# Attention and mixture of experts in one kernel: tile pairs of neighbouring tokens, first products moved into the attention's tail, second-layer tiles issued in pairs

## The reference

```python
scores = scale * np.matmul(q, k.transpose(0, 1, 3, 2))
x = (log1p(abs(i - j)) / log1p(max(i, 1)))[..., None]
bias = np.maximum(x @ w1 + b1, 0.0) @ w2
attn = softmax(scores + bias.transpose(2, 0, 1)[None])
x = np.matmul(attn, v)            # as (2304, 512)
P = np.exp(x @ w_gate - max)
for _ in range(8):
    P /= P.sum(1, keepdims=True) + 1e-09
    P /= P.sum(0, keepdims=True) + 1e-09
    P *= N / E
for e in range(E):
    out += P[:, e:e + 1] * (np.maximum(x @ moe_w1[e], 0.0) @ moe_w2[e])
```

## Time and profile before

| | before |
|---|---|
| median of 3 runs | 1900.03 us (1897.21 to 1900.62) |
| the profiled execution's own time | 1902.45 us |
| its span | 1900.7 us, mean granted clock 0.992 |
| PE busy | 1862.4 us (98%) |
| PEld / DVE / ACT / POOL busy | 1604.4 / 1069.7 / 769.3 / 1156.8 us |
| chain that ended last | PE 91%, DVE 4%, POOL 3%, issue 1% |

### The profile page before, as it was taken

How to read it: one execution, slowest core, us unless ns; L and a number is a source line. 1 busy time by engine, 2 the same in 40 slices (tenths; PEclk the granted TensorE clock), 3 DMA queues, 4 the chain that set the end, 5 groups by cost and what they waited for, 6 DMA issues and landing times.

```text
span 1900.7 us, 27972 instructions
## 1 busy us (share of the span) xinstructions
PE 1862.4 (98%) x10255; PEld 1604.4 (84%) x10255; DVE 1069.7 (56%) x1844; ACT 769.3 (40%) x1314; POOL 1156.8 (61%) x722
## 2 busy tenths in 40 slices
PE   8899999899899999999999999999999999999999
PEld 4677777588799888988898889888888988888888
DVE  8777777648645554457455544554465445544554
ACT  8777767433233333334333333333333333333331
POOL 7523225367666666666677666666666666666662
PEclk9999999899999999999999999999999999999999
DMA  7663551011122111111211111111121111111110
...
DMA packets 44164, 152.58 MB, mean 80 GB/s; under 512 B 9594, under 2 KB 18042, under 8 KB 29710
## 3 DMA queue, kind: packets, MB, share of 16 engines
...
...
## 4 chain that ended last, share of the span: by engine, by line
PE 91%; DVE 4%; POOL 3%; issue 1%; ACT 0%; DMA 0%; SPq 0%; DVEq 0%; POOLq 0%
PE banks L630 14%; PE banks L629 14%; PE banks L628 13%; PE banks L604 12%; PE banks L602 12%; PE banks L606 12%; PE banks L513 4%; PE banks L474 3%; PE banks L456 3%; POOL qk_hi L1167 3%; PE banks L457 2%; PE banks L539 1%; DVE x_lo L1004 1%; DVE h_lo L1081 1%; DVE total L1066 0%
## 5 line engine op out<-in xcount | busy, mean ns | idle before, releaser
L1194 POOL TENSOR_TENSOR w_lo<-stage,w_hi 128x1024 fp32r<-128x1024 f32 (+1 forms) x288 | 641.4, 2228 | 498.0 <-ACT w_hi L782 497.2
L602 PE MATMUL banks<-x_hi,w_hi 128*128 128x384 f32 x1344 | 452.2, 336 | 12.7 <-DVE u L1074 6.6
L630 PE MATMUL banks<-w_hi,h_lo 128*128 128x512 f32 x1152 | 458.4, 398 | 0.0
L629 PE MATMUL banks<-w_lo,h_hi 128*128 128x512 f32 x1152 | 455.9, 396 | 0.0
L604 PE MATMUL banks<-x_lo,w_hi 128*128 128x384 f32 x1344 | 454.2, 338 | 0.0
L606 PE MATMUL banks<-x_hi,w_lo 128*128 128x384 f32 x1344 | 450.7, 335 | 0.0
L628 PE MATMUL banks<-w_hi,h_hi 128*128 128x512 f32 x1152 | 448.5, 389 | 0.0
L820 ACT ACTIVATE h_hi<-corner 128x384 fp32r<-128x384 f32 x288 | 151.3, 525 | 691.5 <-DVE corner L1074 691.5
L1081 DVE SCALAR_TENSOR_TENSOR h_lo<-corner,h_hi 128x384 fp32r<-128x384 f32 x288 | 338.2, 1175 | 3.1
L1074 DVE TENSOR_TENSOR corner<-u,banks 128x384 f32<-128x384 f32 x288 | 158.3, 550 | 270.7 <-PE banks L606 270.3
L602 PEld LDWEIGHTS banks<-x_hi,w_hi 128*128 128x128 f32 x1344 | 254.0, 189 | 39.0 <-DVE x_lo L1004 9.7
...
## 6 DMA issues: line engine op xcount, KB each, us to landing
...
```

What stands on the lines that cost most here:

```text
L602: pe.matmul(dst, hi[:, w, f], x_hi[:, k, c, :], start=fresh and c == 0, stop=False, skip_group_check=not fresh)
L629: pe.matmul(dst, h_hi[:, g % 2, f, tokens], lo[:, f], start=False, stop=False)
L630: mm = pe.matmul(dst, h_lo[:, g % 2, f, tokens], hi[:, f], start=False, stop=fp == FPAIRS - 1 and f == 1)
L1194: pool.tensor_tensor(lo, of, hi.bitcast(F32), ALU.subtract).then_inc(w_split, 1)
```

## The change

- `x_block` takes tile 2p and its neighbour 2p + 1, so that the first pair is tokens 0 to 767; `out_rows` and `tile_weight` follow. `PIECES_0` falls from 45 to 42.
- ACT makes the rounded inputs of the first pair in the last attention steps (after steps 16, 18 and 19 of the last period and tail steps 0 to 3), and DVE their splits after steps 17 and 19, tail steps 0 to 2, and two behind the tail. ACT's rounding of group 1's weights gets a wait for the last values product. The last period of DVE's loop is written out.
- PE issues products 0 and 1 of group 0 after tail steps 0 and 4.
- The first `split_pair` goes from POOL to DVE, behind the bias stage's last instruction; ACT rounds its input after four bias tiles instead of before them; DVE's two copies for the second piece go behind attention steps 0 and 1. `qk_hi` and `k_lo` become separate tensors per slot, and the buffers of the expert stage get another order in memory (`x_lo` in two tensors).
- Second-layer tiles are issued as `TILES_AFTER`: 0 and 1 after product 1, 2 and 3 after product 3, 4 after product 5, 5 after product 6.
- `scale_first` runs one tile at a time in the `add_tile` places of group 7, not six in a row behind group 6; in a group before a new tile pair, the third combination (`corner[:, 2]`) comes ahead of `split_factor(p + 1, 2)`.

```diff
@@ -45,7 +45,10 @@
 ALL = TILE_PAIRS * PERIODS
 PRODUCTS = ((0, 0, True), (4, 1, True), (1, 0, False), (5, 1, False), (3, 0, True), (2, 1, True), (6, 0, False))
 NP = len(PRODUCTS)
+TILES_AFTER = ((), (0, 1), (), (2, 3), (), (4,), (5,))
+TAIL_PRODUCTS = {(0, 0): 0, (0, 1): 4}
 SUMS = 4
+EARLY = 3
 BLOCK = 2 * P
 RAW = 4 * BLOCK + 2 * DM
 STAGE = RAW + SUMS * BLOCK
...
@@ -132,8 +135,10 @@
             probs_t = eb("probs_t", [P, 2 * KC + 1, S])
             heads = eb("heads", [P, 2, S])
             raw = eb("raw", [P, 2, 2, 2, S])
-            qk_hi = eb("qk_hi", [P, 2, 2, 2, S], F32R)
-            k_lo = eb("k_lo", [P, 2, 2, S], F32R)
+            qk_hi, k_lo = [], []
+            for i in range(2):
+                qk_hi.append(eb(f"qk_hi{i}", [P, 2, 2, S], F32R))
+                k_lo.append(eb(f"k_lo{i}", [P, 2, S], F32R))
             bias = eb("bias", [P, QC, 2, S])
             v_main = eb("v_main", [P, 2, KC, 2 * D])
             v_rest = eb("v_rest", [P, 2, 2 * D])
...
@@ -221,7 +230,7 @@
 
         X_PIECES = PAIRS * B
         LAST = PAIRS * STEPS
-        PIECES_0 = PIECES * (X_PIECES - 1)
+        PIECES_0 = PIECES * (X_PIECES - 2)
         Y_BANK = 2
         LOGIT_BANK = Y_BANK + 3
         TURNED_BANK = Y_BANK + 5
...
@@ -253,7 +262,7 @@
 
         def x_block(p, half, part):
 
-            return x[:, 2 * half:2 * half + 2, part * (N // 2) + p * T:part * (N // 2) + p * T + T]
+            return x[:, 2 * half:2 * half + 2, (2 * p + part) * T:(2 * p + part) * T + T]
 
         def x_sum(p, i):
 
...
@@ -385,7 +397,7 @@
             pairs_of(PAIRS - 1, True)
 
 
-            out_rows = out.rearrange("(a t j p) d -> a t p j d", a=2, t=TILE_PAIRS, p=P)
+            out_rows = out.rearrange("(t a j p) d -> a t p j d", a=2, t=TILE_PAIRS, p=P)
             for g in range(2, ALL):
                 sp.wait_ge(w_split, NW * (g - 1))
                 load_weights(g)
...
@@ -562,10 +574,6 @@
             with pe.Fori(1, PAIRS) as hp:
                 for s in range(STEPS):
                     step(hp, s)
-            for s in range(TAIL):
-                step(PAIRS, s)
-
-
             def product(g, k):
 
                 w, which, fresh = PRODUCTS[k]
...
@@ -573,6 +581,8 @@
                 if g % PERIODS == 0:
                     pe.wait_ge(x_split, NP * p + k + 1)
                 if k == 0:
+                    if g == 0:
+                        pe.wait_ge(biased, 2 * LAST)
                     pe.wait_ge(w_split, NW * g + 2)
                     if g > 0:
                         pe.wait_ge(combined, 5 * g - 1)
...
@@ -601,11 +611,17 @@
                     f = slice(c * P, c * P + P)
                     pe.matmul(dst, hi[:, w, f], x_hi[:, k, c, :], start=fresh and c == 0, stop=False,
                               skip_group_check=not fresh)
-                    pe.matmul(dst, hi[:, w, f], x_lo[:, k, c, :], start=False, stop=False,
+                    pe.matmul(dst, hi[:, w, f], x_low(k)[:, c, :], start=False, stop=False,
                               skip_group_check=not fresh)
                     mm = pe.matmul(dst, lo[:, w, f], x_hi[:, k, c, :], start=False, stop=c == 1,
                                    skip_group_check=not fresh)
                 mm.then_inc(product_done, 1)
+
+            for s in range(TAIL):
+                step(PAIRS, s)
+                for (g, k), after in TAIL_PRODUCTS.items():
+                    if after == s:
+                        product(g, k)
 
             def second_layer(g, j):
 
...
@@ -681,10 +697,11 @@
                 for k in range(NP):
                     if g == 1 and k == 2:
                         turn_logits()
-                    if g < ALL:
+                    if g < ALL and (g, k) not in TAIL_PRODUCTS:
                         product(g, k)
-                    if g > 0 and k > 0:
-                        second_layer(g - 1, k - 1)
+                    if g > 0:
+                        for j in TILES_AFTER[k]:
+                            second_layer(g - 1, j)
                 if g == 0:
                     logits()
 
...
@@ -714,16 +731,16 @@
             def round_pair(n, slot, h):
 
                 act.wait_ge(raw_in[slot], 16 * (n - slot + 2))
-                act.activation(qk_hi[:, slot, :, h, :], raw[:, slot, :, h, :], ACT.Copy).then_inc(rounded, 1)
+                act.activation(qk_hi[slot][:, :, h, :], raw[:, slot, :, h, :], ACT.Copy).then_inc(rounded, 1)
 
             for m in range(AHEAD):
                 hidden_units(m, m, again=False)
-            for h in range(2):
-                round_pair(0, 0, h)
             act.wait_ge(shift_kept, 2)
             for m in range(ROUND):
                 hidden_units(m + AHEAD, (m + AHEAD) % ROUND, again=m + AHEAD >= ROUND)
                 keep_bias(m, m, again=False)
+            for h in range(2):
+                round_pair(0, 0, h)
             with act.Fori(1, BIAS_TILES // ROUND - 1) as i:
                 for slot in range(ROUND):
                     hidden_units(ROUND * i + slot + AHEAD, (slot + AHEAD) % ROUND)
...
@@ -772,6 +789,8 @@
 
                 if i == 0:
                     act.wait_ge(w_in[g % 2], 16 * (g // 2 + 1))
+                    if g == 1:
+                        act.wait_ge(pv_done, len(PV_PARTS) * X_PIECES)
                     if g > 1:
                         act.wait_ge(product_done, NP * (g - 1))
                 elif i == 1:
...
@@ -781,17 +800,11 @@
                 hi, _, of = weight_part(g, i)
                 act.activation(hi, of, ACT.Copy).then_inc(w_rounded, 1)
 
-            for s in range(STEPS):
-                step(PAIRS - 1, s, last=True)
-                if s in (7, 9, 14):
-                    round_weights(0, (7, 9, 14).index(s))
-            for s in range(TAIL):
-                step(PAIRS, s)
-
             def round_factor(p, k):
 
                 if p == 0:
-                    act.wait_ge(scores_ready, 2 * LAST)
+                    act.wait_ge(scores_ready, 2 * (LAST - QC))
+                    act.wait_ge(split_done, 2 * X_PIECES)
                     act.wait_ge(scaled, PIECES_0)
                 else:
                     act.wait_ge(product_done, NP * (PERIODS * p - 1) + k + 1)
...
@@ -799,6 +812,17 @@
                 if needed:
                     act.wait_ge(x_summed, SUMS * p + needed)
                 act.activation(x_hi[:, k], x_factor(p, k), ACT.Copy).then_inc(x_rounded, 1)
+
+            for s in range(STEPS):
+                step(PAIRS - 1, s, last=True)
+                if s in (7, 9, 14):
+                    round_weights(0, (7, 9, 14).index(s))
+                for k in {16: (0,), 18: (1,), 19: (2,)}.get(s, ()):
+                    round_factor(0, k)
+            for s in range(TAIL):
+                step(PAIRS, s)
+                if s < NP - EARLY:
+                    round_factor(0, EARLY + s)
 
             def keep_first(g):
                 act.wait_ge(product_done, NP * g + 1)
...
@@ -838,8 +862,6 @@
                 for j in range(2):
                     act.activation(to[:, :, 4 + j, :], second[:, :, C * j:C * j + E], ACT.Copy).then_inc(logit_ready, 1)
 
-            for k in range(NP):
-                round_factor(0, k)
             for g in range(ALL):
                 p, at = g // PERIODS, g % PERIODS
                 more = g + 1 < ALL
...
@@ -916,9 +938,11 @@
 
             dve.wait_ge(attn_consts_in, 32)
             dve.tensor_copy(select_r[:], select_in).then_inc(select_kept, 1)
-            for h in range(2):
-                dve.wait_ge(raw_in[1], 32)
-                dve.tensor_copy(qk_hi[:, 1, :, h, :], raw[:, 1, :, h, :]).then_inc(rounded, 1)
+            dve.wait_ge(rounded, 2)
+            dve.tensor_tensor(qk_hi[0][D:2 * D, 0, :, :], raw[D:2 * D, 0, 0, :, :],
+                              qk_hi[0][D:2 * D, 0, :, :].bitcast(F32), ALU.subtract).then_inc(split_done, 1)
+            dve.tensor_tensor(k_lo[0][:, :, :], raw[:, 0, 1, :, :], qk_hi[0][:, 1, :, :].bitcast(F32),
+                              ALU.subtract).then_inc(split_done, 1)
 
             def keep_heads(hp, s, half):
 
...
@@ -990,19 +1014,31 @@
                             dve.tensor_copy(probs_t[:, 2 * KC, q_at:q_at + rows],
                                             rest_bank[:, 0:rows]).then_inc(kept_t[2], 1)
 
+            def split_factor(p, k):
+                dve.wait_ge(x_rounded, NP * p + k + 1)
+                if p == 0 and k == EARLY:
+                    dve.wait_ge(scores_ready, 2 * LAST)
+                dve.tensor_tensor(x_low(k), x_factor(p, k), x_hi[:, k].bitcast(F32),
+                                  ALU.subtract).then_inc(x_split, 1)
+
             for s in range(STEPS):
                 step(0, s)
-            with dve.Fori(1, PAIRS) as hp:
+                if s < 2:
+                    dve.wait_ge(raw_in[1], 32)
+                    dve.tensor_copy(qk_hi[1][:, :, s, :], raw[:, 1, :, s, :]).then_inc(rounded, 1)
+            with dve.Fori(1, PAIRS - 1) as hp:
```

(33 more changed lines are left out.)

21 lines of the change are left out of this document (12 added, 9 removed).

## The result

The changed kernel takes 1875.91 us in the median of 4 runs (1874.68 to 1877.17), against 1899.87 before; the ratio is 0.9876, 95% interval 0.9859 to 0.9894. The profiled execution took 1877.03 us with a span of 1874.8 and a mean granted clock of 0.997 (before: 1902.45, 1900.7 and 0.992). The two spans differ by 25.9 us.

| start of, us | before | after | won so far |
|---|---|---|---|
| first score | 65.47 | 61.67 | 3.8 |
| score of step 20 | 132.66 | 129.48 | 3.2 |
| score of step 75 | 330.26 | 325.66 | 4.6 |
| score of step 79 | 347.62 | 345.43 | 2.2 |
| logits (end of group 0's products) | 378.37 | 366.14 | 12.2 |

What follows compares the result with a forecast made beforehand. PE, busy 98%, was taken as the bound. Six parts sum to 22.0 us, giving 1880.4 against the profiled 1902.45 and 1878 against the median of the runs; range 1869 to 1888.

Steps and rivals of the forecast that it cites:

- Part 1: Start: first split on DVE lets PE begin at about 61.5 us; 3.6 us won, bounds 2.5 to 5.
- The clock that might have stayed full: Start: PE, idle some 2 us instead of 5, might keep its clock; up to 1.5 us more.
- Part 2: Attention's tail: early inputs and two products in PE's gaps bring the logits sooner; 8.5 us won, bounds 5.5 to 10.5.
- Part 3: Groups 5 and 6: product 4's later deadline removes both `h_lo` waits; 2.3 us won, bounds 1 to 2.3.
- Part 4: Group 7: spreading the six scalings removes most of the wait for `u`; 5.6 us won, bounds 3 to 6.5.
- the rule: Shared DVE/GpSimd port lock: if four of six scalings block 2.2 us, Part 4 keeps 1 to 3 us of loss.
- rival A: DVE and POOL collisions, with four scalings blocked 2.2 us each, eat more: gain 14, time 1886 us; chance 0.17.
- Part 5: New tile pairs, groups 32 and 64: most of the `h_lo` wait stays; 2 us won, bounds 0 to 6.3.
- rival B: Clock stays full, no half-clock stretch left in the tail and at group 64: 1870 to 1873 us; chance 0.14.
- C: Steady groups: product 6 waits for the corner, 0.5 us in each of 96 groups, giving 1926 us; chance 0.04.
- D: Tail inputs late, products 0 and 1 hold PE up: Part 2 wins 2 us, time 1884 to 1885; chance 0.08.
- Part 6: Steady groups: product 6's corner deadline gets tighter but 1.6 us is left; nothing won or lost, 96 times.

Runs made afterwards that it cites:

- e3: The changed kernel with the first split of queries and keys on GpSimd again: 1879.49 us, ratio 0.9900.
- e2: The changed kernel with the six scalings again in one row behind group 6: 1882.54 us, ratio 0.9923.
- e5: The changed kernel with products 0 and 1 of group 0 issued behind the tail: 1874.58 us, ratio 0.9887.
- e6: The changed kernel with the third corner again behind the third input split before a new tile pair: 1876.00 us, ratio 0.9895.
- e8: e7 with DVE's small cast behind the first split, and input splits 5 and 6 moved in the tail and at new tile pairs: 1868.13 us, ratio 0.9852.
- e10: e9 with products 0 and 1 of group 0 issued behind the tail: 1875.49 us, ratio 0.9891.
- e12: e8 with the third input split behind the third hidden split at a new tile pair: 1869.03 us, ratio 0.9849.
- e1: The kernel before with only the second-layer tiles issued in pairs: 1893.62 us, ratio 0.9973.
- e7: The changed kernel with GpSimd's group 0 weight splits and input sums waiting for DVE's last-but-one inverse chain: 1870.69 us, ratio 0.9864.
- e11: e5 with the first pair's inputs rounded and split behind the tail: 1882.73 us, ratio 0.9924.
- e4: The changed kernel with one second-layer tile behind each of products 1 to 6 again: 1883.61 us, ratio 0.9922.
- e9: e8 with the third input split behind the third hidden split, and splits 5 and 6 placed as in the changed kernel: 1874.78 us, ratio 0.9879.

## Why the prediction was right, and where it wasn't

The time lies 2.1 us from the forecast, but partly by luck, since terms missed in opposite directions.

| term | predicted us | from the trace |
|---|---|---|
| 1, start, to step 20 | 3.6 (2.5 to 5) | 3.2 |
| attention steps 20 to 79 | none | +1.4, then -2.4 |
| 2, tail, last score to logits | 8.5 (5.5 to 10.5) | 10.05 |
| 3, routing groups | 2.3 (1 to 2.3) | 2.0 |
| 4, scalings | 5.6 (3 to 6.5) | 6.6 |
| 5, new tile pairs | 2 (0 to 6.3) | 5.0 |
| 6, steady groups | 0 | 0.00 |
| sum | 22.0 | 25.9 |

The last column sets two single executions side by side, and that of the kernel before took 1902.45 us, 2.6 more than the median. The medians differ by 24.0 us, the ratio gives 23.6, both between the sum forecast and the sum of the traces.

Part 1: the first score was said for 61.5 and came at 61.67. The size was right, the cause only for two thirds: e3 shows 1.4 us for the two casts that no longer hold GpSimd off, which I had counted only as a cost. The pipeline then gave back 0.6 (0.4 said). The clock that might have stayed full ("up to 1.5 more") did so in other kernels with this start: PE is at half clock from 63.7 to 67.1 in the changed kernel's trace and at no time there in e2, e5, e6, e8, e10 and e12, and in all of these but e5 step 20 comes 66.5 us behind the first score instead of 67.8 (66.9 in e5).

Between steps 20 and 75 the forecast had nothing, and 1.4 us were won. Of these 0.9 lie between steps 60 and 65, which take 18.59 us before, 18.73 in e1 and 17.73 in the changed kernel and e2 to e12. What those share, and the first two lack, is DVE's last period, the one that starts at step 60, written out of its loop; that this is the cause was not tested alone.

The term that was missing: I had the sums on GpSimd "right behind its weight splits" and took it as a gain for the tail's cast, which it was (that cast is 0.17 us in the tail now). I didn't ask what else DVE does just then. The chain of the piece before meets them, and the wait there grew from 2.17 to 3.5 us with twice the time at half clock, 2.4 us in all between these two traces (e1's trace, without any stretch at half clock there, takes 15.78 us from step 75 to step 79, the kernel before 17.36 and the changed one 19.77). The view that shows it was open: the cast's maximum of 2.04 in the earlier trace rows is that of this very place, at 334.40, and not of the last piece, whose cast took 1.55. e7 proves the cause.

Part 2: the mechanism, early inputs, is right (e11). The size is right by luck. My walk took its start, 24.2 us, from a trace with 13.7 us at half clock in the tail; against e1's trace of the same tail the gain is 5.6 us, at the lower bound of 5.5, and against e11's 6.1. The wait for `u` came as said, 1.9 for 2.5, and the stretch ran at full clock, worth the 1.6 that I had put aside. Wrong is what I credited to product 0 in the first idle stretch: e5 is no slower without it. In my walk the gap ended up in front of product 3, which is a wait moved and not one removed.

Part 3: 2.0 of 2.3; the rest is a new wait of 0.43 us at L693, ahead of product 1 of group 5. The column sums were ready in time, at 434.73 for 438.19, as I had said. What PE waits for is the third corner of group 4, which is due there too and which I left out: before, it ended at 448.93, 0.85 us ahead of its use, less than the 1.39 that the deadline moved up. Part 4: all but nothing was left of the loss, and of the rule's four scalings of six blocked for 2.2 us (rival A) there was one: DVE's timeline of group 7 has the third at 2.15 us, two at 0.73 and 0.96 and the other three at 0.48:

```profile
476.64 0.73 DVE L1102 TENSOR_SCALAR total<-total,routing 128x512 f32<-128x512 f32 x1
...
477.75 2.15 DVE L1102 TENSOR_SCALAR total<-total,routing 128x512 f32<-128x512 f32 x1
...
480.97 0.48 DVE L1102 TENSOR_SCALAR total<-total,routing 128x512 f32<-128x512 f32 x1
```

The blocking that the Trainium skill states (SBUF — State Buffer, "SBUF: two separate sides") is there in this row, in the cast of 2.04 us and in e12; what the count of chances didn't tell is whether somebody waits.

Part 5 is the term that was furthest off, 2 us for 5.0. I had said that DVE's row of work begins 1.39 later too and stays "nearly without a gap from there. So most of the wait stays". Product 4's wait of 2.33 us went altogether, and one of 0.64 us at second-layer tile 0 came. DVE's three input splits do begin 1.4 us later in group 32 (6.2 instead of 4.8 us behind its start), but GpSimd's weight split, which waits for ACT and so for product 2, begins 2.3 later (8.5 instead of 6.2); the three are nearly through by then and take 3.21 instead of 5.40 us. e1 and e4 give 1.2 to 1.7 us a tile pair to the tile order, e6 0.5 to the corner, and the half clock behind group 64's wait went with it, 1.6. e9 shows how thin this is: the row back at 5.40 and the wait back at 2.35.

Of rival B (1870 to 1873) the clock gains in the tail and at group 64 did come, and the new half-clock stretch ahead of the tail took much of it back. Rivals C and D are refuted, C by the 15.640 us and D by the tail. One part of D was right: in this kernel the two products in the tail win nothing (e5). Part 6 stands: 15.640 us a group in both kernels, where my sum of blocks made it 15.69.
